# A fused attention and expert kernel: one wait of ScalarE moved, one TensorE loop rotated, the last matmuls reordered

## The chip, the core and the metric

The kernel runs on one core of a Trainium2 chip. A core has five engines with queues of their own: TensorE (PE in the profile, with PEld for its weight loads), VectorE (DVE), ScalarE (ACT), GpSimd (POOL) and SyncE (SP, which here issues transfers). They meet through semaphores. Each engine has a sequencer that reads the instructions, computes register values, takes branches, and hands the engine its work in order; the profile marks rows of a sequencer with a q (PEldq is TensorE's). The metric is the device time of one execution in microseconds (us); less is better.

## What is computed

The reference, cut to what matters:

```python
# attention: softmax over a band |i-j| < 4, plus a softmax over 4-fold pooled q, k, v; B,H,S,D = 4,8,576,64
x = (out_up + out_local).transpose(0, 2, 1, 3).reshape(2304, 512)
# one expert of eight for each token
logits = x @ w_gate                       # 512 x 8
for e in range(8):                        # tokens whose argmax is e
    h = np.maximum(x[mask] @ w1[e], 0.0)  # 512 x 1024
    out[mask] = gate_w[mask, None] * (h @ w2[e])   # 1024 x 512
# a dense layer pair over all tokens
h = out @ w_in                            # 512 x 2048
g = np.where(h >= 1, h, np.where(h <= -1, 0.0, (h + 1) ** 2 / 4))
return g @ w_out                          # 2048 x 512
```

## The kernel before

There are three stages one behind another: the attention (to about 200 us), the expert stage (to about 498 us) and the dense stage (to the end). Every fp32 product of the last two stages is made of three matmuls on a high and a low part of each operand (`three`, L1301 to L1305), so the profile shows them as L1303, L1304 and L1305 in turn.

**Expert stage.** Tokens are sorted by expert into slots of 128 rows. There is room for 25 slots (`SLOTS`); how many are used depends on the data, and the number of the last one is read from memory as `end`. In the profiled execution 21 are used, so `end` is 20. For slot s TensorE does four things: `turn_x(s)` transposes the tokens (4 transposes into `sc`), `hidden(s)` is the first layer (24 matmuls into `tp`), `turn_h(s)` transposes the result of relu (8 transposes into `pt`), `project(s)` is the second layer (24 matmuls into `xo`). `weights_of(s)` (L1307 to L1309) lets the sequencer read from a table which expert's weights a slot uses. The loop is pipelined by one slot: a pass of it is `hidden(s)`, `turn_x(s + 1)`, `project(s - 1)`, `turn_h(s)`, and it runs over s = 1 to 23 with the condition `s < end` (L1371, L1372), so the passes from `end` on are skipped one by one by the sequencer. Then comes the last slot (`slot(end, True)`), the transposes of the first tokens of the dense stage (`turn_x2(0, 0, k)`, L1384), and `project(end)`. VectorE copies tokens (`copy_rows`, L1011), splits results in high and low parts (L1015, L1017, L1028, L1030), applies relu (L1022) and scales the output rows of a slot in `xg` (`take_y`, L1034). SyncE stores each slot's rows to `y_rows` (`store_slot`, L401), waits until they have landed, and after the last used slot and four skipped passes of its own raises `all_stored` (L417).

**Dense stage.** It runs over 6 groups of three 128-token tiles. In a group step f goes over 16 pieces of 128 hidden columns: `hidden2(g, par, f)` (12 matmuls into `tp`), and, two steps later, `rows(g, f - 2)` (9 matmuls, three for each token tile, into the banks `sc`, `pt`, `pt`, which add up over f). Between them each step passes VectorE's clamp (L1078), ScalarE's square (L767), VectorE's `act_f` (L1082), ScalarE's rounding to the high part `act_s` (L769) and GpSimd's low part (L571). `hidden2(g, par, f)` waits for `act_f` of step f - 2, since there are two banks `tp`; `rows(g, f)` waits for GpSimd's low part of step f. Steps 2 and 3 of `act_f`, and `rows_out`, lie in memory that `xg` held, so they may be written only behind `all_stored`: VectorE waits for it at the `act_f` of step 2 of group 0, ScalarE ahead of group 0.

**The end of a group.** After the last matmul on a tile ScalarE copies its bank to `rows_out` (`take_group`, L762), and GpSimd scatters the rows to the output with an indirect transfer (`scatter_rows`, L566). In groups 0 to 4 this lies beside the next group's matmuls; in the last one it is the end of the kernel.

The order of each engine's work is the order in which it is written here.

Of the kernel before, what the change touches and what calls it, by code (L numbers as in the profile page):

```python
# [62 lines left out]
GT = 3  # L63
GROUPS = TILES // GT
KFF = FF // P
# [14 lines left out]
def write_program(nc, ctx, q, k, v, w_gate, w1, w2, w_in, w_out, out, x_nat, y_rows):  # L80
# [234 lines left out]
    all_stored = sem("all_stored")  # L315
# [281 lines left out]
    def _(act):  # L597
# [157 lines left out]


        def take_group(g):
            if not (isinstance(g, int) and g == 0):
                act.wait_ge(rows_stored, 16 * GT * g)
            for n in range(GT):  # L760
                act.wait_ge(o_full, GT * g + n + 1)
                act.copy(rows_out[:, n, :], o_ps[n][:]).then_inc(o_evac, 1)  # L762
# [9 lines left out]
            take_group(g)  # L772

        act.sem_inc(o_evac, GT)
        act.wait_ge(all_stored, 1)
        group(0, True)
        with act.Fori(1, GROUPS) as g:
            group(g)
# [321 lines left out]
    def _(pe):  # L1100
# [259 lines left out]
        turn_h(0)  # L1360
        keep_clock(sc[1], SPARE // 2)

        def slot(s, last):
            hidden(s, *weights_of(s))
            if not last:
                turn_x(s + 1)
            project(s - 1, *weights_of(s - 1))
            turn_h(s)

        end = pe.value_load(last_slot, min_val=TILES - 1, max_val=SLOTS - 1)  # L1370
        with pe.Fori(1, SLOTS - 1) as s:  # L1371
            with pe.If(s < end):  # L1372
                slot(s, False)
        slot(end, True)

        def turn_x2(g, par, k):
            first = isinstance(g, int) and g == 0
# [23 lines left out]
                          lambda part: x2T[par][:, part, k, :], k == 0, k == KD - 1)  # L1401
            e.then_inc(h2_full, 1)

        def rows(g, f):
            pe.wait_ge(act_lo, KFF * g + f + 1)
            if isinstance(g, int) and g == 0:
                pe.wait_ge(lo_done, NCH * (E + 1) + f + 1)
            for i in range(GT):
                if f == 0:
                    pe.wait_ge(o_evac, GT * g + i + 1)  # L1410
                e = three(o_ps[i][:], lambda part: act_s[f % 4][:, part, i * P:(i + 1) * P],
                          lambda part: wts[:, 1, part, f * CH:(f + 1) * CH], f == 0, f == KFF - 1)
                if f == KFF - 1:
                    e.then_inc(o_full, 1)

        def group(g, par, last):
            for f in range(KFF + 2):
                if f < KFF:
                    hidden2(g, par, f)
                if f >= 2:  # L1420
                    rows(g, f - 2)
                if not last and 8 <= f < 8 + KD:
                    turn_x2(g + 1, 1 - par, f - 8)

        group(0, 0, False)
        with pe.Fori(0, GROUPS // 2 - 1) as i:
            group(2 * i + 1, 1, False)
            group(2 * i + 2, 0, False)
        group(GROUPS - 1, 1, True)


_INS = ["q", "k", "v", "moe_w_gate", "moe_w1", "moe_w2", "moe2_w_in", "moe2_w_out"]
# [19 lines left out]
```

## Time and profile before

| | |
|---|---|
| median of 3 runs | 918.72 us (917.51 to 921.9) |
| the profiled execution | 921.8 us, of which the trace spans 919.9 us |
| TensorE busy in the span | 871.2 us (95%) |
| VectorE, ScalarE, GpSimd busy | 447.7, 369.2, 450.2 us |
| mean granted TensorE clock | 0.982 of full speed |

The span runs from the first to the last instruction of the trace; 1.9 us of the execution's time lie around it. Rows of the timeline begin with the start and the length in us. A bracket behind a row is the idle time of the engine ahead of it and what ended it. Matmuls are pipelined, so their lengths overlap; the time that one costs is the distance to the next one's start.

### The profile page before, as it was taken

Reading aid. Unit: us, or ns where it says so; the run is one execution under the profiler, and the core shown is the slowest. Engines: PE = TensorE matmul, PEld = TensorE weight load, DVE = VectorE, ACT = ScalarE, POOL = GpSimd, SP = SyncE. Lnnn points to the kernel's source line nnn. Section 1 sums busy time; section 2 is a strip of 40 time slices with the busy share of each in tenths; the row PEclk is TensorE's granted clock in tenths of the full one; section 3 lists DMA queues with packets and bytes.
Section 4 is the critical chain, followed back from the end, with each engine's and each line's share of the span. In section 5 each row is a group of like instructions: output and inputs, shape, how many; then the busy total and the mean of one; then the engine's idle time right before and its main releaser. Section 6 shows DMA issues by size and latency. Waiting matters only on the chain.

```text
span 919.9 us, 17885 instructions
## 1 busy us (share of the span) xinstructions
PE 871.2 (95%) x5190; PEld 750.4 (82%) x5191; DVE 447.7 (49%) x1192; ACT 369.2 (40%) x1013; POOL 450.2 (49%) x470
## 2 busy tenths in 40 slices
PE   6999999956998999999998999999999999999995
PEld 5878888845785888888877998999989999899995
DVE  3888888866554545554544242242242242242221
ACT  5888888841322443234222423323223223223222
POOL 4556555665987886588444631421422322322322
PEclk9999999986999999999999999999999999999998
DMA  7355666444776665466434200100200100200000
GB/s 159 78 136 139 148 146 167 116 120 115 217 231 170 197 197 163 128 199 205 137 115 119 101 1 1 70 1 0 70 1 1 69 0 0 69 0 0 35 1 35
DMA packets 109992, 88.71 MB, mean 96 GB/s; under 512 B 67904, under 2 KB 81728, under 8 KB 109952
## 3 DMA queue, kind: packets, MB, share of 16 engines
q10 hardware_dynamic: 23040, 41.95, 15.4%
q1 hardware_dynamic: 83472, 34.87, 14.5%
q0 software_dynamic: 3440, 11.38, 3.9%
q8 instruction: 22, 0.36, 0.2%
q14 instruction: 18, 0.15, 0.0%
HBM read 73.07 MB, written 15.10 MB: 96 GB/s over the span
## 4 chain that ended last, share of the span: by engine, by line
PE 85%; POOL 5%; DMA 3%; issue 3%; DVE 2%; ACT 1%; SPq 0%; ACTq 0%; POOLq 0%; DVEq 0%
PE tp L1303 10%; PE tp L1305 10%; PE tp L1304 10%; PE sc L1138 5%; PE pt L1305 5%; PE pt L1304 5%; PE pt L1303 5%; PE xo L1303 4%; PE xo L1305 3%; PE xo L1304 3%; POOL wts L466 3%; PE tp L1215 3%; PE sc L1304 2%; PE sc L1305 2%; PE sc L1303 2%
## 5 line engine op out<-in xcount | busy, mean ns | idle before, releaser
L571 POOL TENSOR_TENSOR act_s<-act_f,act_s 128x384 fp32r<-128x384 f32 x96 | 97.4, 1015 | 285.5 <-ACT act_s L769 285.4
L466 POOL TENSOR_TENSOR wts<-stage,wts 128x512 fp32r<-128x512 f32 x160 | 205.3, 1306 | 64.7 <-ACT wts L675 58.8
L675 ACT CAST wts<-stage 128x512 fp32r<-128x512 f32 x160 | 98.5, 621 | 206.6 <-DMA stage<-in_moe_w 90.9
L1078 DVE TENSOR_SCALAR clamped<-tp 128x384 f32<-128x384 f32 x96 | 53.5, 558 | 195.9 <-PE tp L1305 195.9
L767 ACT ACTIVATE clamped<-clamped,mhalf 128x384 f32<-128x384 f32 x96 | 59.2, 617 | 217.8 <-DVE clamped L1078 208.4
L1303 PE MATMUL tp<-x2T,wts 128*128 128x384 f32 x384 | 132.1, 344 | 2.7 <-DVE act_f L1082 2.7
L1305 PE MATMUL tp<-x2T,wts 128*128 128x384 f32 x384 | 129.8, 338 | 0.0
L1304 PE MATMUL tp<-x2T,wts 128*128 128x384 f32 x384 | 129.5, 337 | 0.0
L1082 DVE SCALAR_TENSOR_TENSOR act_f<-tp,clamped 128x384 f32<-128x384 f32 x96 | 53.5, 558 | 68.9 <-ACT clamped L767 68.9
L1303 PEld LDWEIGHTS tp<-x2T,wts 128*128 128x128 f32 x384 | 72.6, 189 | 6.5 <-DVE act_f L1082 3.0
L1303 PE MATMUL tp<-wts,xT 128*128 x168 | 68.7, 409 | 7.6 <-POOL wts L466 4.9
L1305 PE MATMUL pt<-wts,act_s 128*128 128x512 f32 x192 | 75.8, 395 | 0.0
L1304 PE MATMUL pt<-wts,act_s 128*128 128x512 f32 x192 | 75.5, 393 | 0.0
L1304 PEld LDWEIGHTS tp<-x2T,wts 128*128 128x128 f32 x384 | 72.7, 189 | 2.8
L1303 PE MATMUL pt<-wts,act_s 128*128 128x512 f32 x192 | 74.5, 388 | 0.0
L616 ACT ACTIVATE prob<-prob,nmax 96x112 f32<-96x112 f32 x192 | 71.8, 379 | 4.0 <-DVE nmax L809 2.9
L769 ACT CAST act_s<-act_f 128x384 fp32r<-128x384 f32 x96 | 49.3, 514 | 59.9 <-DVE act_f L1082 59.9
L1305 PEld LDWEIGHTS tp<-x2T,wts 128*128 128x128 f32 x384 | 72.6, 189 | 0.0
L1303 PE MATMUL xo<-wts,hT 128*128 x168 | 67.5, 402 | 2.1 <-issue 1.6
L1304 PE MATMUL tp<-wts,xT 128*128 x168 | 66.2, 394 | 0.0
L1305 PE MATMUL tp<-wts,xT 128*128 x168 | 66.1, 394 | 0.0
L1305 PE MATMUL xo<-wts,hT 128*128 x168 | 65.7, 391 | 0.0
(187 smaller groups left out, 1678.0 us busy)
## 6 DMA issues: line engine op xcount, KB each, us to landing
stage<-in_moe_w ACTq DMA_DIRECT2D x128, 256.0 KB, 3.0
y_rows<-xg SPq DMA_DIRECT2D x21, 260.0 KB, 3.5
vw<-in_v SPq DMA_DIRECT2D x96, 56.0 KB
x<-y_rows SPq DMA_DIRECT2D x6, 780.0 KB, 4.5
qn<-in_q SPq DMA_DIRECT2D x32, 144.0 KB, 3.3
kn<-in_k SPq DMA_DIRECT2D x32, 144.0 KB, 3.2
v<-in_v SPq DMA_DIRECT2D x16, 288.0 KB
x_nat<-xb SPq DMA_DIRECT2D x16, 288.0 KB, 4.0
```

Of the source, the lines that this page charges most:

```text
L466: pool.tensor_tensor(wts[:, par, 1, cols], stage[:, n % STG, :], wts[:, par, 0, cols], ALU.subtract).then_inc(lo_done, 1)
L571: pool.tensor_tensor(act_s[f % 4][:, 1, :], act_f[f % 4][:], act_s[f % 4][:, 0, :], ALU.subtract).then_inc(act_lo, 1)
L616: e = act.activation(prob[par][g][:, i, :], prob[par][g][:, i, :], ACT.Exp, bias=nmax[par][:, 3 * g + i:3 * g + i + 1], scale=-1.0, accum_ ...
L675: act.copy(wts[:, par, 0, n * CH:(n + 1) * CH], stage[:, n % STG, :]).then_inc(hi_done, 1)
L767: act.activation(clamped[f % 2][:], clamped[f % 2][:], ACT.Square, bias=mhalf[:], scale=0.5).then_inc(square_done, 1)
L769: act.copy(act_s[f % 4][:, 0, :], act_f[f % 4][:]).then_inc(act_hi, 1)
L1078: dve.tensor_scalar(clamped[f % 2][:], src, -1.0, 1.0, ALU.max, ALU.min).then_inc(clamp_done, 1)
L1082: dve.scalar_tensor_tensor(act_f[f % 4][:], src, -1.0, clamped[f % 2][:], ALU.max, ALU.add).then_inc(act_done, 1)
L1138: e = pe.matmul(sc[g % 2][0:TQ, i * W:(i + 1) * W], qT[par][D * hh:D * hh + D, TQ * t:TQ * t + TQ], kT[par][D * hh:D * hh + D, WSTART[t]:W ...
L1303: pe.matmul(o, stationary(0), moving(0), start=start, stop=False)
L1304: pe.matmul(o, stationary(1), moving(0), start=False, stop=False)
L1305: return pe.matmul(o, stationary(0), moving(1), start=False, stop=stop)
```

## The change

Three edits. ScalarE's wait for `all_stored` goes from the start of group 0 to its first copy into `rows_out`, at the end of group 0. TensorE's expert loop is rotated: `hidden(1)` stands ahead of it, a pass is `turn_x(s + 1)`, `project(s - 1)`, `turn_h(s)`, `hidden(s + 1)`, and `project(end - 1)` and `turn_h(end)` stand behind it. In the last group of the dense stage the last 18 matmuls are in another order.

```diff
@@ take_group(g), ScalarE @@
-            if not (isinstance(g, int) and g == 0):
+            if isinstance(g, int) and g == 0:
+                act.wait_ge(all_stored, 1)
+            else:
                 act.wait_ge(rows_stored, 16 * GT * g)
@@ ScalarE, ahead of group 0 @@
         act.sem_inc(o_evac, GT)
-        act.wait_ge(all_stored, 1)
         group(0, True)
@@ TensorE, expert loop @@
-        def slot(s, last):
-            hidden(s, *weights_of(s))
-            if not last:
-                turn_x(s + 1)
-            project(s - 1, *weights_of(s - 1))
-            turn_h(s)
-
         end = pe.value_load(last_slot, min_val=TILES - 1, max_val=SLOTS - 1)
+        hidden(1, *weights_of(1))
         with pe.Fori(1, SLOTS - 1) as s:
             with pe.If(s < end):
-                slot(s, False)
-        slot(end, True)
+                turn_x(s + 1)
+                project(s - 1, *weights_of(s - 1))
+                turn_h(s)
+                hidden(s + 1, *weights_of(s + 1))
+        project(end - 1, *weights_of(end - 1))
+        turn_h(end)
@@ rows, TensorE @@
-        def rows(g, f):
+        def rows(g, f, tiles=range(GT)):
-            for i in range(GT):
+            for i in tiles:
@@ group, TensorE @@
-                if f >= 2:
+                if f >= 2 and not (last and f >= KFF):
                     rows(g, f - 2)
@@ behind the last group @@
         group(GROUPS - 1, 1, True)
+        rows(GROUPS - 1, KFF - 2, (0, 1))
+        rows(GROUPS - 1, KFF - 1, (0,))
+        rows(GROUPS - 1, KFF - 2, (2,))
+        rows(GROUPS - 1, KFF - 1, (1, 2))
```

The sequencer's view of TensorE's loop. Before, the end of a pass: the last matmuls of `project`, the transposes `turn_h` (L1343), the loop's end (L1371, L1372), and then the table reads for `hidden` (L1308, L1309).

```order
L1303 MATMUL xo<-wts,hT 128x512
L1304 MATMUL xo<-wts,hT 128x512
L1305 ISA
L1305 MATMUL xo<-wts,hT 128x512
L1338 REGISTER_ALU
L1340 REGISTER_ALU
L1343 MATMUL pt<-ident,hs 128x128 x8
L1372 UNCONDITIONAL_BRANCH
L1371 REGISTER_ALU
L1371 COMPARE_AND_BRANCH
L1308 ISA
L1308 TENSOR_LOAD tables
```

The same loop's end in the changed kernel, where all lines are one further down or more (L1366, L1367 are the loop, L1309, L1310 the table reads), followed by what comes after the last pass.

```order
L1305 MATMUL tp<-wts,xT 128x512
L1306 ISA
L1306 MATMUL tp<-wts,xT 128x512
L1367 UNCONDITIONAL_BRANCH
L1366 REGISTER_ALU
L1366 COMPARE_AND_BRANCH
L1309 ISA
L1309 TENSOR_LOAD tables
L1309 ISA x2
L1310 ISA
L1310 TENSOR_LOAD tables
L1310 ISA x2
```

The loop's end stood behind 24 matmuls of `project` and 8 transposes, and stands now behind the 24 matmuls of `hidden`; behind the last pass the table reads are those of `project(end - 1)`. TensorE's matmuls and transposes keep their order.

ScalarE at the start of the dense stage, before, with its waits:

```order
L670 DMA stage<-in_moe_w_out 128x512 [waits lo_done]
L675 CAST wts<-stage 128x512 [waits stage_loaded3]
L767 ACTIVATE clamped_183<-clamped_183,mhalf 128x384 [waits clamp_done,all_stored]
L769 CAST act_s_187<-act_f_186 128x384 [waits act_done]
L670 DMA stage<-in_moe_w_out 128x512 [waits lo_done]
```

And in the changed kernel:

```order
L670 DMA stage<-in_moe_w_out 128x512 [waits lo_done]
L675 CAST wts<-stage 128x512 [waits stage_loaded3]
L769 ACTIVATE clamped_183<-clamped_183,mhalf 128x384 [waits clamp_done]
L771 CAST act_s_187<-act_f_186 128x384 [waits act_done]
L670 DMA stage<-in_moe_w_out 128x512 [waits lo_done]
```

The square of step 0 no longer waits for `all_stored`; VectorE's wait for it at step 2 is unchanged.

TensorE's last matmuls, before (`act_s2` is step 14, `act_s3` step 15; `sc0`, `pt0`, `pt1` are token tiles 0, 1, 2):

```order
L1303 MATMUL pt0<-wts_56,act_s2_189 128x512
L1304 MATMUL pt0<-wts_56,act_s2_189 128x512
L1305 MATMUL pt0<-wts_56,act_s2_189 128x512
L1303 MATMUL pt1<-wts_56,act_s2_189 128x512
L1304 MATMUL pt1<-wts_56,act_s2_189 128x512
L1305 MATMUL pt1<-wts_56,act_s2_189 128x512
L1303 MATMUL sc0<-wts_56,act_s3_190 128x512
L1304 MATMUL sc0<-wts_56,act_s3_190 128x512
L1305 MATMUL sc0<-wts_56,act_s3_190 128x512
```

The same nine places in the changed kernel:

```order
L1304 MATMUL pt0<-wts_56,act_s2_189 128x512
L1305 MATMUL pt0<-wts_56,act_s2_189 128x512
L1306 MATMUL pt0<-wts_56,act_s2_189 128x512
L1304 MATMUL sc0<-wts_56,act_s3_190 128x512
L1305 MATMUL sc0<-wts_56,act_s3_190 128x512
L1306 MATMUL sc0<-wts_56,act_s3_190 128x512
L1304 MATMUL pt1<-wts_56,act_s2_189 128x512
L1305 MATMUL pt1<-wts_56,act_s2_189 128x512
L1306 MATMUL pt1<-wts_56,act_s2_189 128x512
```

Tile 0 gets its last three matmuls ahead of tile 2's step 14; the last six matmuls, tiles 1 and 2 of step 15, stand where they stood.

## Rows read from the trace of the kernel before

**Rows 1.** Stretches: length, busy us of PE PEld DVE ACT POOL, PEclk, DMA share, GB/s

```profile
230.00:296.00 66.00, 59.85 (x286) 47.10 (x284) 34.15 (x52) 17.27 (x28) 54.96 (x49) 1.00 0.72 205
474.10:498.00 23.90, 21.63 (x102) 17.73 (x101) 12.11 (x20) 4.87 (x8) 10.07 (x8) 0.93 0.38 111
512.00:906.00 394.00, 394.00 (x2007) 356.36 (x2006) 125.86 (x226) 116.07 (x205) 116.63 (x119) 1.00 0.06 21
```

**Rows 2.** Timeline, PE where the expert loop ends

```profile
474.08 1.03 PE L1343 MATMUL pt<-ident,hs 128*128 128x128 f32 x8
476.96 0.49 PE L1303 MATMUL tp<-wts,xT 128*128 x1 [1.84 <-issue]
...
484.18 0.39 PE L1303 MATMUL xo<-wts,hT 128*128 x1
```

**Rows 3.** Lines L1371, L1309, sequencer, loop's end: ns min/median/max, first and last start

```profile
L1371 PEldq ALU_OP  x5: 32/36/36, 471.8 to 474.8; - x5
...
L1309 PEldq SEQ_ASSERT  x1: 18/18/18, 476.5 to 476.5; - x1
```

**Rows 4.** Timeline of an ordinary pass, PE and DVE

```profile
446.71 0.39 PE L1305 MATMUL xo<-wts,hT 128*128 x1
...
448.99 1.03 PE L1343 MATMUL pt<-ident,hs 128*128 128x128 f32 x8
...
449.77 0.48 PE L1303 MATMUL tp<-wts,xT 128*128 x1
...
452.78 0.65 DVE L1011 COPY xs<-xg 128x512 f32 x1
...
455.32 0.60 PE L1320 MATMUL sc<-ident,xs 128*128 128x128 f32 x4
```

**Rows 5.** Lines L1371, L1318, sequencer, in that pass

```profile
L1371 PEldq ALU_OP  x1: 32/32/32, 446.7 to 446.7; - x1
...
L1318 PEldq EVENT_SEMAPHORE  x1: 51/51/51, 451.9 to 451.9; - x1
```

**Rows 6.** Timeline, PE at the loop's start

```profile
233.25 0.49 PE L1303 MATMUL tp<-wts,xT 128*128 x1 [1.48 <-POOL wts L466]
```

**Rows 7.** Timeline, start of the dense stage, all engines

```profile
500.36 0.56 DVE L1078 TENSOR_SCALAR clamped<-tp 128x384 f32<-128x384 f32 x1 [1.29 <-PE tp L1305]
...
501.99 0.34 PE L1305 MATMUL tp<-x2T,wts 128*128 128x384 f32 x1
...
503.75 0.61 ACT L767 ACTIVATE clamped<-clamped,mhalf 128x384 f32<-128x384 f32 x1 [9.36 <-SPq L417]
504.40 0.56 DVE L1082 SCALAR_TENSOR_TENSOR act_f<-tp,clamped 128x384 f32<-128x384 f32 x1 [3.48 <-ACT clamped L767]
...
505.01 0.62 PE L1303 MATMUL tp<-x2T,wts 128*128 128x384 f32 x1 [2.68 <-DVE act_f L1082]
...
505.58 1.01 POOL L571 TENSOR_TENSOR act_s<-act_f,act_s 128x384 fp32r<-128x384 f32 x1 [9.81 <-ACT act_s L769]
...
508.59 0.33 PE L1305 MATMUL tp<-x2T,wts 128*128 128x384 f32 x1
508.76 0.40 PE L1303 MATMUL sc<-wts,act_s 128*128 128x512 f32 x1
```

**Rows 8.** Line L401, the stores of the slots

```profile
DMA to landing us min/median/max: 2.1/3.5/4.3
```

**Rows 9.** Timeline, the end of the kernel, all engines

```profile
906.79 1.01 POOL L571 TENSOR_TENSOR act_s<-act_f,act_s 128x384 fp32r<-128x384 f32 x1 [3.17 <-ACT act_s L769]
...
908.75 0.39 PE L1305 MATMUL sc<-wts,act_s 128*128 128x512 f32 x1
...
909.17 0.59 ACT L762 COPY rows_out<-sc 128x512 f32<-128x512 f32 x1 [2.46 <-PE sc L1305]
...
910.59 1.01 POOL L566 DMA_INDIRECT out_rows<-rows_out,tok_i  x1 [2.78 <-ACT rows_out L762]
...
913.17 0.97 POOL L566 DMA_INDIRECT out_rows<-rows_out,tok_i  x1 [0.30 <-issue]
```

## The prediction

> **What bounds the kernel now.** I read first the busy times by stretch [rows 1]. From 512 to 906 us TensorE is busy for all of its 394.00 us at full clock, so in the dense stage only fewer matmuls would help, and the change removes none. Two stretches stand out: in 474 to 498 us TensorE is busy 21.63 of 23.90 us at a granted clock of 0.93, and around 505 us it stands idle once more. These are the places of the first two edits; the third works on the last microseconds. Next come the timeline of TensorE there and the rows of its sequencer, since an idle stretch with "issue" behind it has no other engine to blame.
>
> *The loop's end.* The transposes of slot 19 start at 474.08 [rows 2]. In an ordinary pass the next first layer starts 0.78 us behind such transposes (448.99 to 449.77) and takes 5.55 us to the work behind it (449.77 to 455.32) [rows 4]. So the last first layer could start at 474.86 and the projection behind it at 480.41. It starts at 476.96, behind 1.84 us of "issue", and the projection at 484.18 [rows 2]. The loss is 484.18 - 480.41 = 3.77 us: 2.10 us of late start and 1.67 us of slow matmuls (7.22 us for what takes 5.55). The granted clock of 0.93 in this stretch says why they are slow: TensorE ran at 1.2 instead of 2.4 GHz for a part of it, right behind the idle time. The late start is the sequencer's: it adds one to s five times, from 471.8 to 474.8 (four passes that are skipped, and the exit), and ends its table reads at 476.5 [rows 3].
>
> *The start of the dense stage.* The clamp of step 0 is done at 500.36 + 0.56 = 500.92, but ScalarE's square starts at 503.75, released by SyncE's `all_stored` behind 9.36 us [rows 7]. VectorE's `act_f` follows at 504.40, and TensorE, which needs it for the third `hidden2`, starts at 505.01 behind 2.68 us of idle time. Its 12 matmuls then last until 508.76, 3.75 us; at the full clock one costs 0.17 us (508.59 to 508.76), so 12 cost 2.1. The first eleven steps are 0.33 us apart, again about half the rate behind an idle stretch.
>
> *The end.* GpSimd's low part of step 15 ends at 906.79 + 1.01 = 907.80. Tile 0's last matmul starts at 908.75, its copy at 909.17, the first scatter at 910.59 and the third at 913.17 [rows 9]. The three scatters run back to back on GpSimd, 1.29 us apart, so the first one sets when the third one ends.
>
> **Edit 1, ScalarE's wait.** Nothing that ScalarE writes ahead of its new wait lies under `xg`; VectorE still waits at step 2. Square 0 starts when the clamp is done, at 500.92 + 0.04 = 500.96. From there to TensorE's start the rows give 505.01 - 503.75 = 1.26 us, so `act_f` 0 releases the third `hidden2` at 502.22. TensorE has issued the second one by 501.99 + 0.17 = 502.16. The idle time shrinks from 2.7 us to below 0.1, and with it I expect the slow stretch to go: 502.22 + 2.1 = 504.3, against 508.76. I take **4.4 us**.
>
> What is late next? `rows(0, 0)` then wants the low part of step 0. Today GpSimd starts it at 505.58, 0.62 us behind the end of `act_f` (504.96), for 1.01 us [rows 7]; moved, it ends at 502.2 + 0.6 + 1.0 = 503.8, before 504.3. VectorE's `act_f` of step 2, which keeps the wait, would be due at about 504.5 (clamp) + 0.6 + 0.7 = 505.8. `all_stored` is there at 503.7, so 2 us are spare. The store that raises it can land later: between 2.1 and 4.3 us over the 21 slots [rows 8]. Even with 2.2 us more VectorE would be late by 0.2 us, and TensorE asks for that result only at the fifth `hidden2`, behind two `rows` and a `hidden2`. The new wait, behind step 15 of group 0, is met long before. Queued behind the old wait were ScalarE's weight copies for the second layer (pieces 8 to 15), which now start earlier; they are wanted from step 8 on.
>
> **Edit 2, the rotated loop.** The work of the sequencer is the same, its place is not. At the loop's start `hidden(1)` has a little less ahead of it. That gives nothing: it waited there for GpSimd's low part (1.48 us) [rows 6], which doesn't move. Within the loop the edge moves from behind `turn_h` to behind `hidden`. There the sequencer comes to `turn_x` at 451.9 today [rows 5], and VectorE's copy of the tokens ends only at 452.78 + 0.65 = 453.43 [rows 4], so 1.5 us of slack cover the edge. I put both at nothing.
>
> At the loop's end the four skipped passes now stand behind `hidden(20)`. How much of it is still to be executed when the sequencer gets there? In the ordinary pass it reaches the edge at 446.7 [rows 5], while TensorE runs the 15th of 24 matmuls (446.71; the transposes start at 448.99, and a matmul costs 5.55 / 24 = 0.23 us) [rows 4]: 9 matmuls and 8 transposes ahead, 17 in all. At the end of `hidden` (451.9) it is (455.32 - 451.9) / 0.23 = 15 matmuls ahead. In the changed loop the reads for `hidden(20)` follow `turn_h(19)` without an edge, so the lead is larger than in that pass; I take 17. They cost 17 x 0.23 = 3.9 us of TensorE, so the edge comes at 480.41 - 3.9 = 476.5. From the edge to the end of the table reads the last pass needs 476.5 - 471.8 = 4.7 us [rows 3], and to the first matmul another 0.45 (476.96). The projection then starts at 476.5 + 4.7 + 0.45 = 481.65, 1.24 us late instead of 3.77. A first matmul behind a gap costs 0.1 us more than one in a row, which today's at 484.18 is not. I take **2.4 us**; with a lead of 15 it is 2.0, and if the sequencer is held by its own speed alone 2.6.
>
> This assumes the full clock behind the new gap. It is 1.2 us long. In the stretch 230 to 296 us the gap of 1.48 us [rows 6] left the clock at 1.00 [rows 1]; the gap of 1.84 us did not. The new gap is on the good side of both, not by much.
>
> Everything behind it (the transposes, the last projection, the store, `all_stored`) moves with it, so edit 1's sum keeps its distances. ScalarE's loads for the second layer wait for `hidden(20)` and start earlier as well.
>
> **Edit 3, the last matmuls.** Tile 0's step 15 starts at 908.75 - 2 x 0.23 = 908.3 now. Three matmuls (0.7 us) ahead of it go behind it, so it could start at 907.6; the low part is there only at 907.80, so it starts at 907.85 and TensorE stands 0.25 us. Tile 0's last matmul is at 907.85 + 0.45 = 908.3 instead of 908.75, its copy, the first scatter and with it the third 0.45 us earlier. Tile 2's copy comes 0.25 us later, at about 910.8, and its scatter is due at 913.17 - 0.45 = 912.7, so that costs nothing. I take **0.4 us**; the ends are 0, if the first scatter waits for something else, and 0.45.
>
> **Sum.** 4.4 + 2.4 + 0.4 = 7.2 us. The span goes from 919.9 to 912.7 us, the profiled execution from 921.8 to 914.6. It was the slowest of its kind: the median is 918.72, 3.1 us lower. The three terms are idle time and half-rate stretches at fixed places, not shares of the time, so I take them off the median too: 918.72 - 7.2 = **911.5 us**, 0.8% less.
>
> **Rivals.**
> *The clock drops behind the new gap.* Then 1.67 us are lost again [rows 2], the gain is 5.5, the time 913.2. For it: 1.2 us is not far from 1.48, and only one such gap was seen to be harmless. Chance 0.15.
> *Edit 1 takes away only the wait.* A slow stretch comes at the same place or a little later, or a step of the chain through ScalarE is late behind its weight copies. The gain of edit 1 is then 2.7, the whole 5.5, the time 913.2. Against it: no idle time above 0.1 us is left for the drop to follow. Chance 0.08. With both, 914.9: 0.04.
> *The rotated loop pays at each edge.* This one ends on the slow side. If the edge is not covered, each of 19 passes pays for it, in the loop and not once. A skipped pass, which is an edge and little else, takes the sequencer (474.8 - 471.8) / 4 = 0.75 us [rows 3]; 19 of them make 14.3 us, a time of 918.72 - 7.2 + 14.3 = 925.8. The gain is gone from 7.2 / 19 = 0.38 us a pass on. Against it stands the slack of 1.5 us ahead of `turn_x`: an edge would have to take 1.9 us. Chance 0.03.
> The Trainium skill names a cause of such a thing. By Runtime: NRT & Kernel Launch, section Instruction fetch mechanics, a taken branch to a target outside the part of the program that has been fetched stalls the sequencer until that part is there. If the new edge fell so, the time would be that of this rival or above. The trace does not bear it out at the old edge: the four skipped passes, each with its jump, cost 0.75 us each and no more.
> *The change doesn't show.* The two stalls may differ between executions, as the spread of 917.5 to 921.9 suggests, or be smaller than in the profiled one. A gain below 4.6 us remains. Chance 0.08.
>
> **How the numbers follow.** The forecast of 7.2 us has 0.62 (with the bounds of the terms, 6.0 to 8.0 us, so 910.7 to 912.7). The two at 913.2 add 0.23. A measurement of this kernel can tell about 0.5% (4.6 us) from no change, so faster means below 914.1. Faster: 0.62 + 0.23 and a small part of the fourth case, 0.86. Within 0.5%: both drops together and the rest of the fourth, 0.11. Slower: 0.03. The range reaches to the cases at 913.2 with the spread of the medians, 909.0 to 914.4.
>
> **What the profile after would show.** Edit 1: ScalarE's first square about 0.05 us behind the first clamp, no idle time of TensorE above 0.1 us between the first two `hidden2` and the third, full clock there. Edit 2: the "issue" gap no longer behind the transposes but behind the last `hidden`, 1.0 to 1.5 us long, followed by matmuls 0.23 us apart; the sequencer's five additions start about 4.7 us later than `turn_h(19)` was issued. The passes of the loop keep their length. Edit 3: a gap of about 0.25 us ahead of tile 0's last three matmuls, and the first scatter 0.4 us earlier, counted from the low part of step 15. I am wrong if the passes of the loop get longer, if the clock falls behind the new gap, or if VectorE's step 2 waits for `all_stored` long enough to hold TensorE.

## The result, and the profile after

| | |
|---|---|
| median, changed kernel | 915.18 us (8 runs) |
| median, kernel before, same chip | 920.96 us (8 runs) |
| ratio | 0.9943, 95% interval 0.9928 to 0.9958 |
| profiled execution after | 915.04 us, its trace spans 913.1 us |
| predicted | 911.5 us (909.0 to 914.4); profiled execution 914.6, span 912.7 |

The kernel is faster by 5.3 us (3.9 to 6.6, from the ratio and 920.96; the two medians lie 5.8 apart), where 7.2 were predicted. One execution of each kernel ran slowly (932.76 and 936.62 us); both medians include it, the ratio leaves both out. The profiled execution came out within 0.4 us of its forecast; that agreement is partly luck: between the two profiled executions the attention, which is not touched, got 1.4 us shorter, and the expert loop 1.8 us longer, as the table of stages shows.

The head of the page after: span, then busy time, share and instructions of each engine.

```profile
span 913.1 us, 17866 instructions
...
PE 868.4 (95%) x5190; PEld 747.3 (82%) x5191; DVE 449.6 (49%) x1192; ACT 369.3 (40%) x1013; POOL 449.6 (49%) x470
```

TensorE is busy 2.8 us less than the 871.2 before, though it executes the same matmuls: slow ones are gone. The busy times by stretch of after (length, busy us of PE, PEld, DVE, ACT, POOL, granted clock, DMA share, GB/s), which answer to [rows 1]:

```profile
474.00:498.00 24.00, 22.72 (x117) 19.02 (x116) 12.86 (x21) 4.87 (x8) 10.10 (x8) 1.00 0.37 111
498.00:512.00 14.00, 14.00 (x73) 12.79 (x72) 5.02 (x9) 6.97 (x13) 8.99 (x8) 1.00 0.48 151
512.00:902.00 390.00, 389.92 (x1984) 352.11 (x1983) 124.37 (x223) 114.36 (x203) 113.45 (x116) 1.00 0.06 20
```

The clock of the first stretch is 1.00 in place of 0.93, and TensorE is busy for all of 498 to 512 us.

Timeline of all engines at the start of the dense stage, after (start, length, engine, line; answers to [rows 7]):

```profile
498.23 0.56 DVE L1079 TENSOR_SCALAR clamped<-tp 128x384 f32<-128x384 f32 x1 [1.28 <-PE tp L1306]
498.82 0.62 ACT L769 ACTIVATE clamped<-clamped,mhalf 128x384 f32<-128x384 f32 x1 [7.86 <-DVE clamped L1079]
499.48 0.56 DVE L1083 SCALAR_TENSOR_TENSOR act_f<-tp,clamped 128x384 f32<-128x384 f32 x1 [0.69 <-ACT clamped L769]
...
502.28 0.39 PE L1304 MATMUL sc<-wts,act_s 128*128 128x512 f32 x1
```

The square starts 0.03 us behind the end of the clamp (498.23 + 0.56 = 498.79), released by the clamp and not by `all_stored`. TensorE shows no idle time ahead of the first `rows` at 502.28.

Timeline of TensorE where the expert loop ends, after, answering to [rows 2]:

```profile
480.66 0.39 PE L1306 MATMUL tp<-wts,xT 128*128 x1
481.92 0.49 PE L1304 MATMUL xo<-wts,hT 128*128 x1 [0.87 <-issue]
```

The additions of its sequencer there, after (ns min/median/max, first and last start), answering to [rows 3]:

```profile
L1366 PEldq ALU_OP  x5: 32/36/36, 476.8 to 479.8; - x5
```

And the end of its table reads for `project(end - 1)`, after:

```profile
L1310 PEldq SEQ_ASSERT  x1: 18/18/18, 481.5 to 481.5; - x1
```

The gap stands now behind `hidden(20)` and is 0.87 us long in place of 1.84; the five additions still take 3.0 us.

The end of the kernel after, all engines, answering to [rows 9]:

```profile
900.27 1.01 POOL L571 TENSOR_TENSOR act_s<-act_f,act_s 128x384 fp32r<-128x384 f32 x1 [3.17 <-ACT act_s L771]
...
901.34 0.50 PE L1304 MATMUL sc<-wts,act_s 128*128 128x512 f32 x1
...
902.35 0.59 ACT L764 COPY rows_out<-sc 128x512 f32<-128x512 f32 x1 [2.16 <-PE sc L1306]
...
903.76 1.01 POOL L566 DMA_INDIRECT out_rows<-rows_out,tok_i  x1 [2.48 <-ACT rows_out L764]
...
905.13 0.97 POOL L566 DMA_INDIRECT out_rows<-rows_out,tok_i  x1 [0.37 <-ACT rows_out L764]
...
906.41 0.97 POOL L566 DMA_INDIRECT out_rows<-rows_out,tok_i  x1 [0.30 <-issue]
```

From the start of the low part to the third scatter it is 906.41 - 900.27 = 6.14 us, against 6.38 in [rows 9].

**Where the time went, by stages.** One trace of each kernel is too few here, since stages that the change does not touch differ between traces too. So the table holds twelve further traces, told of below: three of these same two kernels, and nine of variants. "Attention" ends with its last transposes; "passes" are the 14 passes of the expert loop behind the second expert's weights, between two projections; "loop's end" goes from there to the first transposes for the dense stage; "step 0" from the first `hidden2` to `rows(0, 0)`; "tail" from the low part of step 15 to the third scatter. Times in us.

| trace | attention | to the passes | passes | loop's end | step 0 | tail |
|---|---|---|---|---|---|---|
| before | 195.79 | 99.80 | 172.92 | 21.97 | 10.79 | 6.38 |
| before, again | 194.05 | 99.31 | 173.12 | 21.99 | 10.75 | 6.38 |
| before, third | 194.82 | 100.14 | 173.33 | 22.00 | 10.73 | 6.38 |
| old loop, ScalarE's wait moved | 195.00 | 100.28 | 173.51 | 22.00 | 6.45 | 6.38 |
| the same and the last matmuls | 194.87 | 100.66 | 173.30 | 20.35 | 6.45 | 6.11 |
| old loop, a read more in a pass | 194.47 | 100.47 | 173.61 | 20.39 | 10.77 | 6.38 |
| rotated loop alone | 195.01 | 100.01 | 173.76 | 19.41 | 11.03 | 6.38 |
| after | 194.41 | 99.85 | 174.74 | 19.39 | 6.43 | 6.14 |
| after, again | 194.07 | 100.94 | 174.21 | 19.37 | 6.45 | 6.11 |
| third place for the loop's edge | 194.13 | 100.10 | 172.71 | 20.23 | 6.43 | 6.11 |
| reads ahead of the loop (e9) | 195.62 | 100.82 | 175.34 | 18.21 | 6.44 | 6.12 |
| reads ahead of the loop (e12) | 195.36 | 100.88 | 173.21 | 18.23 | 6.45 | 6.12 |
| thin low parts, old loop | 194.86 | 97.07 | 172.29 | 22.00 | 10.76 | 6.38 |
| thin low parts, rotated loop | 193.75 | 97.27 | 173.99 | 19.38 | 10.59 | 6.38 |

Three things can be read off. Step 0 is 4.3 us shorter wherever the wait is moved, and nowhere else. The rotated loop ends in 19.4 us, the old one in 22.0 or 20.4. And the passes of the rotated loop are longer, where nothing else is changed in them. The attention, which no kernel touches, ends anywhere between 193.75 and 195.79 us; 1.4 of the 6.8 us between the spans of the two profiled executions are of that kind. The 175.34 of e9 and the 173.99 of the thin low parts with the rotated loop hold a first pass of 13.9 us with slow matmuls in it, told of below.

### The profile page after: what moved, and what is told of

The parts are those of the page before. It is cut to its first block, busy times and chain, and to the rows that moved or that the text cites. A ratio compares the mean times of both kernels' runs of the same rounds, so it can differ in the third digit from the quotient of the medians.

```text
span 913.1 us, 17866 instructions
## 1 busy us (share of the span) xinstructions
PE 868.4 (95%) x5190; PEld 747.3 (82%) x5191; DVE 449.6 (49%) x1192; ACT 369.3 (40%) x1013; POOL 449.6 (49%) x470
## 4 chain that ended last, share of the span: by engine, by line
PE 85%; POOL 5%; DMA 3%; issue 3%; DVE 2%; ACT 1%; SPq 0%; ACTq 0%; POOLq 0%; DVEq 0%
PE tp L1304 10%; PE tp L1306 10%; PE tp L1305 10%; PE sc L1139 5%; PE pt L1306 5%; PE pt L1305 5%; PE pt L1304 5%; PE xo L1304 4%; PE xo L1306 3%; PE xo L1305 3%; POOL wts L466 3%; PE tp L1216 3%; PE sc L1305 2%; PE sc L1306 2%; PE sc L1304 2%
## 5 line engine op out<-in xcount | busy, mean ns | idle before, releaser
L466 POOL TENSOR_TENSOR wts<-stage,wts 128x512 fp32r<-128x512 f32 x160 | 205.2, 1304 | 63.3 <-ACT wts L675 57.8
```

What stands on the lines that cost most here:

```text
L466: pool.tensor_tensor(wts[:, par, 1, cols], stage[:, n % STG, :], wts[:, par, 0, cols], ALU.subtract).then_inc(lo_done, 1)
```

## The experiments

### The parts of the change by themselves

The edits are the hunks of the diff above: e1 has the loop alone, e2 the two hunks of ScalarE, e3 those and the last matmuls, e4 is the changed kernel once more.

> Only TensorE's expert loop is rotated. The changed kernel's profile has the loop's end 2.7 us cheaper, but the 14 passes between the first projection behind the weights (295.59 before, 294.26 after) and the last one (468.52, 468.99) cost 1.8 us more. Theory 1 (the new edge ahead of turn_x costs in the passes, in every execution): the gain is about 2.7 - 1.8 = 0.9 us, and the passes of this trace are 1 to 2 us longer than those of before. Theory 2 (the 1.8 us are chance, slow token copies of VectorE that met GpSimd's low parts): the gain is about 2.6 us, and the passes are now longer, now shorter.

> Only ScalarE's wait for all_stored is moved. Predicted 4.4 us; the changed kernel's trace shows 4.35 us between the start of the dense stage and the first rows. Both theories: 4.4 us less time, no idle time of TensorE above 0.1 us ahead of the third hidden2. If the store of the last slot or ScalarE's weight copies came in the way without the rotation, less than 4.

> The wait moved and the last 18 matmuls reordered, the loop as before. The reordering brought 0.24 us in the changed kernel's trace, so 4.6 us less than before. Theory 1: as fast as the changed kernel or nearly (within 1 us), since the rotation gives only 0.9 us net. Theory 2: 2.6 us slower than the changed kernel. The trace is one more sample of the passes with the old edge: 172.9 us from the first to the last projection if they are as before.

> The changed kernel once more, for a second trace and for its ratio beside the other three on one chip. Theory 1: the passes take again about 174.7 us and the gain is 5 to 5.5 us. Theory 2: the passes take about 173 us in this trace and the gain of the profiled execution is nearer to 7.

| | median | ratio to before | 95% interval |
|---|---|---|---|
| e1, loop alone | 919.72 | 0.9979 | 0.9966 to 0.9991 |
| e2, ScalarE's wait alone | 917.22 | 0.9942 | 0.9921 to 0.9964 |
| e3, wait and last matmuls | 916.03 | 0.9938 | 0.9916 to 0.9959 |
| e4, all three | 915.56 | 0.9935 | 0.9916 to 0.9954 |

The wait carries nearly everything. The rotated loop gives 1.9 us alone (0.8 to 3.1), which lies between the 0.9 of the first theory of e1 and the 2.6 of the second, so neither holds as told; and what it adds on top of e3 is less than the intervals. By the ratios e1 and e2 add to 1.9 + 5.3 = 7.2 us and e4 gives 6.0; the intervals, 1.1 to 2 us to each side, don't tell these apart, nor from the sum of the stages below.

In e2 and e1 each edit shows its own stage in the table and leaves the other's alone. One exception speaks for the wait: in e1, where the old wait is kept, the slow matmuls behind TensorE's 2.67 us of idle time last 6.83 us in place of 3.41, and some are still slow in the steps that follow, which costs 1 us more there. Stretch of e1 (columns as above):

```profile
501.00:509.00 8.00, 6.35 (x18) 5.85 (x19) 2.70 (x5) 4.09 (x8) 4.45 (x4) 0.57 0.54 165
```

So what the old wait costs is 4.3 us in six of the seven traces that have it and 5.6 in the seventh.

e3 brought the surprise. It has the old loop, and its gap behind `turn_h(19)` is the one of [rows 2], but no matmul behind it is slow. TensorE's timeline, e3:

```profile
477.27 0.49 PE L1304 MATMUL tp<-wts,xT 128*128 x1 [1.84 <-issue]
```

The stretch of it, e3, with the columns as above:

```profile
474.10:498.00 23.90, 21.63 (x110) 18.09 (x110) 12.87 (x21) 4.87 (x8) 10.10 (x8) 1.00 0.34 112
```

The same 1.84 us of idle time, clock 1.00 here and 0.93 in [rows 1]. Behind a gap of this length the clock falls in some executions and not in others.

### How often does the clock fall there?

e10 and e11 are the kernel before, run again for one trace each.

> The kernel before once more, for its trace. In the five traces with the old loop end the gap there was 1.84 to 1.91 us every time, but the clock fell to half behind it in three and stayed full in two. If the fall is chance, this trace shows either; the 2.68 us gap at the start of the dense stage had the fall behind it in all traces that have it, and will here.

> As the run before: one more sample of the half-rate stretch behind the old loop's end, and of the 14 passes (172.9 to 173.6 us with the old edge).

They took 919.78 and 921.62 us. Both had the slow stretch; the row of e10 has the 0.93 again:

```profile
472.00:496.00 24.00, 21.73 (x102) 17.78 (x101) 12.11 (x20) 4.87 (x8) 10.09 (x8) 0.93 0.35 112
```

Over all traces with the old loop's end (gaps of 1.84 to 1.90 us), five had it (22.0 us to the dense stage) and two had not (20.35 and 20.39). The length of the gap does not tell them apart: behind 1.84 us the clock fell in two traces and not in e3, behind 1.90 it fell in e11 and not in e8. What decides it stays open. The rotated loop, with its 0.87 us, never had it: 19.37 to 19.41 us in four traces. The gain at the loop's end is therefore 2.6 us five times in seven and 1.0 us twice, 2.1 us on average.

### Why the passes of the rotated loop are longer

The six old-loop traces with ordinary weights have 172.92 to 173.61 us for the 14 passes, mean 173.30; the three rotated ones 173.76 to 174.74, mean 174.24. I took this for the loop's edge first: that it has less cover in its new place, or that the sequencer stalls there for instructions. The timelines named something else. Most passes take 12.27 us in both loops; the long ones all begin with a slow copy of the tokens by VectorE. A slow pass of after, all engines:

```profile
414.39 6.58 POOL L466 TENSOR_TENSOR wts<-stage,wts 128x512 fp32r<-128x512 f32 x5 [2.20 <-ACT wts L675]
...
415.64 1.58 DVE L1012 COPY xs<-xg 128x512 f32 x1
...
419.24 0.49 PE L1304 MATMUL xo<-wts,hT 128*128 x1 [0.47 <-issue]
```

The copy takes 0.43 us by itself; here it takes 1.58, while GpSimd prepares weights in pieces of 1.3 us (the first row is five of them in a row). The transposes of `turn_x` wait for it, behind that wait the sequencer reads the tables for `project`, and TensorE has run out of queued work by then. Two experiments test the copy against the edge: GpSimd's work is made short in both loops, so that the edge alone is left.

```diff
-        def low_part(c, par, n):
+        def low_part(c, par, n, width=CH):
...
-                    low_part(2 * i + 2 + cc, cc, n)
+                    low_part(2 * i + 2 + cc, cc, n, 16)
```

e6 has this with the old loop, e7 with the rotated one, both without the other two edits. They leave out most of the low part of six experts' weights.

> Leaves out a part of the computation: for six of the eight experts GpSimd computes the low part of the weights for 16 of 512 columns of a chunk only. The loop is that of before. If VectorE's slow token copies (1.1 to 1.6 us instead of 0.43) come from GpSimd's low parts beside them, nearly all copies take 0.43 us and 14 passes cost 171.8 us (12.27 each) instead of 173.2. If the copies are slow for another cause, the passes stay at 173.

> The same part left out, with the rotated loop. If the rotation costs only where a token copy is slow, the passes are 171.8 us here too, and the two kernels differ by the loop's end alone. If the new edge costs something of its own in each pass, they are longer than those of the old loop without GpSimd's low parts.

The copies of the 14 passes in the kernel before (ns min/median/max, first and last start):

```profile
L1011 DVE COPY xs<-xg x14: 427/526/1558, 305.0 to 465.0; 128x512 f32 x14
```

The same of after:

```profile
L1012 DVE COPY xs<-xg x14: 427/568/1581, 303.7 to 465.4; 128x512 f32 x14
```

The same of e6, thin low parts with the old loop:

```profile
L1011 DVE COPY xs<-xg x14: 427/428/1552, 301.3 to 460.8; 128x512 f32 x14
```

The same of e7, thin low parts with the rotated loop:

```profile
L1011 DVE COPY xs<-xg x14: 426/427/1540, 302.0 to 461.5; 128x512 f32 x14
```

With thin low parts the copies take 0.43 us in both loops but for the last, where GpSimd is at the dense stage's weights in full pieces. The passes take 12.27 us in both loops but for the last (12.84 in the old, 12.94 in the rotated one) and the first of e7 (13.86), in which TensorE was slow behind several waits for weights. So the edge in its new place costs nothing where the copy is short; time is lost where the copy is slow, in both loops. The medians were 917.83 us (ratio 0.9967, 0.9952 to 0.9982) and 915.68 (0.9955, 0.9931 to 0.9978); most of what e6 gains lies ahead of the passes (97 us in place of 100).

The Trainium skill has the rule for the copy: by SBUF — State Buffer, section Who interferes with whom, VectorE and GpSimd share a pair of SBUF ports under an exclusive lock, so that an operation which needs it waits until the other engine's instruction is done. The trace agrees. A copy that begins while one of GpSimd's subtractions runs ends 0.28 to 0.29 us behind that subtraction, however long it has still to go. One of each kind, timeline, before:

```profile
390.85 1.31 POOL L466 TENSOR_TENSOR wts<-stage,wts 128x512 fp32r<-128x512 f32 x1
391.17 1.28 DVE L1011 COPY xs<-xg 128x512 f32 x1
```

The subtraction ends at 392.16, the copy at 392.45. It is so for all 118 of the 196 copies (14 in each of the 14 traces) that begin with more than 0.2 us of a subtraction left, and the 73 that begin with none running take 0.43 to 0.47 us. The longest copy is then 1.30 + 0.28 = 1.58 us, as seen, and what makes a copy slow is only where in GpSimd's piece it begins.

**What a slow copy costs in either loop.** In the old loop a pass is longer than 12.27 us by the copy's length less 0.99 (1.28 gives 0.30, 1.56 gives 0.58), in the rotated one by its length less 0.88 (1.25 gives 0.38, 1.58 gives 0.72). The 0.1 us is found in the sequencer's rows. `turn_x` has two waits, for the copy (`xs_done`) and for `xT_done`. In the last pass of before the sequencer has passed `xT_done` at 464.2 (this row), and only the wait for the copy is left, long before the copy ends (465.05 + 1.56 = 466.61), sequencer, before:

```profile
L1318 PEldq EVENT_SEMAPHORE  x1: 51/51/51, 464.2 to 464.2; - x1
```

The table reads follow at once, at 466.7, sequencer, before:

```profile
L1308 PEldq FUSED_REGOPS  x2: 46/98/151, 466.7 to 467.1; - x2
```

The same pass of after has its copy end at 465.43 + 1.55 = 466.98, timeline of VectorE, after:

```profile
465.43 1.55 DVE L1012 COPY xs<-xg 128x512 f32 x1
```

In the old loop `xT_done` is compared with the same value for which `hidden(s)` waited just ahead, and no addition for it is seen. Here the wait for the copy comes first, and the value for `xT_done` is computed only behind it, sequencer, after:

```profile
L1319 PEldq ALU_OP  x1: 32/32/32, 467.0 to 467.0; - x1
```

And the reads start behind it, at 467.1, sequencer, after:

```profile
L1309 PEldq FUSED_REGOPS  x2: 46/98/151, 467.1 to 467.6; - x2
```

The two rules account for the passes of the nine traces to within 0.12 us. Fourteen of 12.27 us make 171.78. With the copies above 1 us (four to six in each) and the excess of each over 0.99 or 0.88 us, the sum is 172.97 for before and 174.67 for after, against 172.92 and 174.74 measured; e1 and e4 come to 173.80 and 174.18, against 173.76 and 174.21. Of the 0.94 us between the means, 0.1 us on each of some five slow passes is 0.5. The other 0.4 is that the copies themselves were slower: counted over 0.99 us they add to 1.19 to 1.83 us in the old-loop traces (mean 1.56) and to 1.58, 1.96 and 2.23 in the rotated ones. Whether the rotation shifts VectorE against GpSimd or this is chance stays open. Two further kernels with a rotated loop, e5 and e12 below, speak for chance: they have 0.89 and 1.43 us there.

### Is there slack for more work of the sequencer?

e8 puts a read of 0.75 us ahead of `turn_x` in the old loop.

```diff
             if not last:
+                pe.value_load(slot_par[0:1, bass.ds(s, 1)], min_val=0, max_val=1)
                 turn_x(s + 1)
```

> The kernel before with one more table read by TensorE's sequencer ahead of turn_x in each pass, about 0.75 us, as long as a skipped pass. If what stands ahead of turn_x is covered by the token copy (the sequencer comes 1.5 us before it), the passes stay at 172.9 to 173.5 us. If time of the sequencer ahead of turn_x costs passes, they grow by up to 14 x 0.75 = 10 us.

921.46 us, ratio 1.0012 (1.0000 to 1.0025), passes 173.61 us, the upper end of the old loop's. Of the 1.5 us of slack that the prediction read from [rows 4, 5] at least 0.75 are there: what stands ahead of the copy's wait is covered. What stands behind it is not covered where the copy is slow, as the 0.1 us of `xT_done` show.

### Better places for the edge and for the last reads

e5 puts the edge ahead of `turn_h`: `hidden(1)`, `turn_x(2)` and `project(0)` stand ahead of the loop, and a pass is

```diff
             with pe.If(s < end):
+                turn_h_before(s)
+                hidden(s, *weights_of(s))
                 turn_x(s + 1)
                 project(s - 1, *weights_of(s - 1))
-                turn_h(s)
-                hidden(s + 1, *weights_of(s + 1))
```

where `turn_h_before(s)` does what `turn_h(s - 1)` does.

> The changed kernel with the loop's edge at a third place: a pass is turn_h(s - 1), hidden(s), turn_x(s + 1), project(s - 1), and the loop ends behind a project. There the sequencer is held by the full queue and nothing of it stands ahead of turn_x. The skipped passes cost 3.2 to 4 us of sequencer, without table reads behind them, and up to 17 matmuls and transposes (3.9 us) lie ahead: a gap of 0 to 0.3 us instead of 1.84 or 0.87. The passes go back to 173.0 to 173.5 us. Theory 3 (the rotation lost 0.1 us in each pass with a slow token copy and gave back the rest; the half-rate stretch at the loop's end comes in some executions only): 1 to 2 us faster than the changed kernel, 7 us less than before. Rival: 5.5 us as the changed kernel, if the passes hang on something else.

Median 914.48, ratio 0.9940 (0.9920 to 0.9959). The loop's end takes 20.23 us, longer than the rotated loop's 19.4, since the reads for `hidden(end)` now stand behind both the skipped passes and `turn_h`. TensorE, e5:

```profile
473.10 1.07 PE L1364 MATMUL pt<-ident,hs 128*128 128x128 f32 x8 [0.41 <-issue]
...
475.28 0.49 PE L1305 MATMUL tp<-wts,xT 128*128 x1 [1.11 <-issue]
```

The passes take 172.71 us, with three slow copies only. A gap of 0 to 0.3 us and 1 to 2 us less than the changed kernel were expected; the gap failed on the reads behind `turn_h`, and in sum e5 is no better than the changed kernel.

e9 and e12 take the table reads of `project(end - 1)` from behind the loop, since they depend on `end` alone, and swap the two waits of `turn_x`; e9 reads ahead of `hidden(1)`, e12 behind it.

```diff
         def turn_x(s):
-            pe.wait_ge(xs_done, s + 1)
             if not (isinstance(s, int) and s == 0):
                 pe.wait_ge(xT_done, s)
+            pe.wait_ge(xs_done, s + 1)
...
         hidden(1, *weights_of(1))
+        behind = weights_of(end - 1)
...
-        project(end - 1, *weights_of(end - 1))
+        project(end - 1, *behind)
```

> The changed kernel with two more edits to TensorE's sequencer. The table reads of project(end - 1) stand ahead of the loop instead of behind it, and in turn_x the wait for xT_done, whose value has to be computed, stands ahead of the wait for the token copy instead of behind it. If the gap behind the last first layer (0.87 us) is the sequencer's four skipped passes plus 1.5 us of reads, it goes to 0; if the 0.1 us a slow pass is the value computed behind the copy's wait, the last pass falls from 12.94 to 12.84. Together 1.0 to 1.5 us less than the changed kernel. Rival: the reads are not what bounds there (a queue or the waits of the projection), the gap stays above 0.5 us and the time within 0.3 us of the changed kernel's.

> As the run with early reads, but the reads for project(end - 1) stand behind hidden(1), ahead of the loop, where 24 matmuls lie ahead of them, instead of ahead of hidden(1), where TensorE stood 2.47 us at 234.04. Expected if that place cost something: the gap ahead of hidden(1) is 0.85 us again, the loop's end 18.2 us as with the early reads, the last pass 12.85 us, and the time 1 to 1.5 us below the changed kernel's and 7 us below before. Rival: the start of the expert stage hangs on GpSimd's weight parts alone, so the move changes nothing there, and the time is that of the early reads.

The gap at the loop's end is gone in both. TensorE, e12:

```profile
481.14 0.39 PE L1306 MATMUL tp<-wts,xT 128*128 x1
481.36 0.39 PE L1304 MATMUL xo<-wts,hT 128*128 x1
```

The loop's end takes 18.2 us, 1.2 less, and with the waits swapped the last pass is back at 12.85, the old loop's length. So are the other slow passes: all five of e12 follow the old loop's rule, and their sum is 173.21 us by it and in the trace. This confirms the 0.1 us of the second wait. In e9 the two reads ahead of `hidden(1)` let TensorE stand 2.47 us at 234 us. The clock fell to half for 3.41 us from 235.1, 1.1 us behind the end of that gap; it fell again, for 6.83 us from 293.2, behind waits for weights such as the other traces have too. The second one is what makes e9's first pass 13.93 us (stretch of e9):

```profile
293.00:301.00 8.00, 7.43 (x22) 5.35 (x21) 2.76 (x4) 4.04 (x7) 7.95 (x7) 0.57 0.65 197
```

In e12, with the reads behind `hidden(1)`, the gap ahead of it is 0.81 us and neither slow stretch is there. The medians are 914.52 (ratio 0.9929, 0.9916 to 0.9943) for e9 and 915.96 (0.9942, 0.9925 to 0.9959) for e12; the latter's gain by the ratio is 5.3 us, where 7 were expected. A gain of 1 us that two traces show at a fixed place is not seen in the time: the stages that nobody touched vary by more. No kernel of these is measurably faster than the changed one.

## Why the prediction was off

Three steps failed: the passes of the loop, put at nothing, cost 0.9 us; the 2.4 us of the loop's end hold a part that comes only in some executions; and the base, the median of three runs, was 1.8 to 2.2 us too low. Edit 3 was 0.15 us less than told.

**Edit 1, right.** Predicted 4.4 us, measured 4.36 between the profiled executions and 4.3 between the others. ScalarE's square starts behind the clamp, no idle time of TensorE is left and no slow matmul. Neither the weight copies queued behind the old wait nor VectorE's wait at step 2 held TensorE (busy 14.00 of 14.00 us from 498 to 512). The rival that the edit takes away the wait alone fell.

**Edit 2, loop's end: the mechanism right, the size partly.** The last matmul of `hidden(20)` starts at 480.66, so the projection was due at 480.89; the sequencer reaches the edge at 476.8, 4.1 us or 18 matmuls ahead, where 17 were taken. From there to the end of the reads it needs 481.5 - 476.8 = 4.7 us, as taken. The projection starts at 481.92, 1.03 us late where 1.24 were predicted, behind a gap of 0.87. The rival that the clock drops behind the new gap fell in all of four traces. What failed is the term itself: "I take 2.4 us" counts 1.67 us of slow matmuls as a thing that happens in each execution. It happened in five of seven. The gain is 2.6 or 1.0, on average 2.1.

**Edit 2, loop's start: a wait misread, at no cost.** The prediction held the 1.48 us ahead of `hidden(1)` [rows 6] for a wait for GpSimd's low part, "which doesn't move". They were the sequencer's: it reads `end`, sets up the loop, and reads the tables for `hidden(1)` until 232.8, and the first matmul follows at 233.25. Sequencer, before:

```profile
L1309 PEldq SEQ_ASSERT  x1: 18/18/18, 232.8 to 232.8; - x1
```

With `hidden(1)` ahead of the loop's set-up the gap is 0.6 us shorter. TensorE, after:

```profile
231.32 0.49 PE L1304 MATMUL tp<-wts,xT 128*128 x1 [0.86 <-issue]
```

It was 1.47 to 1.51 us in all seven traces of the old loop and is 0.79 to 0.86 in the four of the changed loop, and two more reads there made it 2.47 (e9). Nothing of it is gained, as the prediction said: "to the passes" is 100.1 us on average in the six old-loop traces with ordinary weights and 100.3 in the three rotated ones. TensorE waits for GpSimd's weights behind it in either case, at 282 to 295 us.

**Edit 2, passes: "I put both at nothing" failed.** They got 0.94 us longer in sum. The check that the prediction made, 1.5 us of slack ahead of `turn_x`, is right (e8), and an edge in that place costs nothing (e7). It was made in a pass whose copy took 0.65 us [rows 4]. In four to six passes of fourteen the copy takes 1.0 to 1.6 us, since GpSimd works beside it; then TensorE runs out of work before the sequencer is through, and what the sequencer does behind the copy's wait adds to the time. The rotation had put there the value of the `xT_done` wait, 0.1 us. The prediction looked at what stands ahead of the wait and not behind it, and at an ordinary pass and not at the slowest ones. How much of the 0.94 us is the rotation's is shown for 0.5 of it only. It also named "I am wrong if the passes of the loop get longer" as a sign, and that is what happened, by 0.07 us a pass rather than the rival's 0.75. That rival, a jump that stalls at each edge, did not come about; by the rule of the Trainium skill cited with it (Runtime: NRT & Kernel Launch, section Instruction fetch mechanics) a stall needs a target that has not been fetched, and e7's passes, 12.27 us as in the old loop, show none.

**Edit 3, mis-sized: 0.25 us for 0.4.** The step "TensorE stands 0.25 us" came out: the matmul before starts at 900.86 and the next one would be due 0.23 us behind it, at 901.09; it starts at 901.34. But this first matmul behind a gap costs 0.33 us to the next one's start in place of 0.23, which the prediction counted in edit 2 and not here. So ScalarE's copy of tile 0 starts 1.07 us behind the end of the low part in place of 1.37, 0.3 us earlier and not 0.45. And the second scatter now waits for ScalarE's copy of tile 1 (0.37 us of idle time in place of 0.30), so the three scatters no longer run as tightly as in [rows 9].

**The sum** of the stages is then -4.3 - 2.1 + 0.9 - 0.25 = -5.75 us, against -5.3 (3.9 to 6.6) and, in e4, -6.0. The prediction had 7.2.

**The base.** The rest of the miss is in the step "so I take them off the median too". The median of three runs, 918.72, lay 2.2 us below that of the eight runs beside the changed kernel, 920.96. Of the 915.18 - 911.5 = 3.7 us by which the time was missed, 2.2 are the base's, and 1.4 the gain's (7.2 less the 5.8 between the two medians). With the gain by the ratio, 5.3, it is 1.9 of the gain's and 1.8 of the base's; either way about half of the miss is not the change's. The range was drawn around the gain and had hardly any room for a base whose three runs spread over 4.4 us. The rival that the change doesn't show, a gain below 4.6 us, fell by the medians; the lower end of the interval, 3.9, is within it.

## What to carry to other kernels

An idle stretch that ends in slow matmuls has two prices, the gap and what the clock takes behind it; the second may come in only some executions, so read it from several traces before it goes into a sum. Take off a gain of a few us from a median of many runs. When work of a sequencer is moved, look at the slowest passes, not at an ordinary one, and ask what stands behind the wait that ends last: register arithmetic there, down to the computed value of the next wait, went straight into the time here. Where one engine's short copy runs beside another's long operations, look at its longest duration first, since it may set the pace of the loop.

## What the runs showed of the hardware that I had not expected

- **The clock behind a gap.** Behind 1.84 to 1.90 us of idle time TensorE ran at half its rate for 3.41 us afterwards in five traces of seven. Behind 2.67 us it did so in all seven, for 3.41 us in six and 6.83 in one, and behind the other gaps of 2.14 to 2.96 us (e1, e3, e4, e5 at 283 to 284 us, e9 at 234) in all five. Behind single gaps of 1.47 to 1.61 us and of 0.87 us it did not. Behind shorter gaps, 1.24 and 1.14 us, it did where TensorE had waited several times before (clock 0.77 in 288 to 294 us of e7, 0.50 in 294 to 300 us of e9); but a like row of waits in before, at 284 to 296 us, left it at 1.00.
- **VectorE's copy beside GpSimd.** A 128x512 copy within SBUF takes 0.43 us alone. Begun while a subtraction of GpSimd runs (1.3 us), it ends 0.28 us behind it, after up to 1.58 us. A subtraction of GpSimd that begins during a copy is at times longer as well (1.49 us in before at 466 us).
- **Two waits in a row.** With the second wait's value computed behind the first, the sequencer was about 0.1 us later behind the first wait's release than with both values computed ahead.
- **What reads cost.** The two table reads of a projection's weights run from 480.05 to 481.54 us in after, 0.75 us each, as long as a skipped pass. Where they don't stand behind enough queued matmuls they show as "issue" or, as at the loop's start, under the name of another engine whose semaphore came last (1.48 us, "POOL wts L466").
